# Routed experts on one core: TensorE transposes taken out, rows stored by expert, activations turned on VectorE and through DRAM

## What is computed

```python
kv = np.einsum('bhsd,bhse->bhde', k, v)            # 8 x 8 heads, 576 x 64
out = np.einsum('bhsd,bhde->bhse', q, kv)
x = out / sqrt(mean(out * out, -1) + 1e-6) * g_norm  # -> (4608, 512)

h = x @ w_in                                       # 512 -> 2048
x = (np.maximum(h, 0) + alpha * np.minimum(h, 0)) @ w_out

e_idx = np.argmax(x @ w_gate, axis=1)              # one of 8 experts
gate, eom = softmax(x @ w_gate) at e_idx, sigmoid(x @ w_output_gate) at e_idx
for e in range(8):                                 # w1[e] 512x1024, w2[e] 1024x512
    out[mask] = gate * eom * (np.maximum(x[mask] @ w1[e], 0) @ w2[e])
```

## Time and profile before

| | |
|---|---|
| median of 3 runs | 1506.88 us (1506.14 to 1508.6) |
| the profiled execution's own time | 1503.35 us |
| its span | 1501.5 us |
| instructions | 27268 |
| moved by DMA | 104.51 MB, mean 70 GB/s |

### The profile page before, as it was taken

How to read it: one execution, slowest core, us unless ns; L and a number is a source line. 1 busy time by engine, 2 the same in 40 slices (tenths; PEclk the granted TensorE clock), 3 DMA queues, 4 the chain that set the end, 5 groups by cost and what they waited for, 6 DMA issues and landing times.

```text
span 1501.5 us, 27268 instructions
## 1 busy us (share of the span) xinstructions
PE 1471.3 (98%) x8553; PEld 1280.6 (85%) x8554; DVE 723.3 (48%) x1796; ACT 490.8 (33%) x994; POOL 127.3 (8%) x143
## 2 busy tenths in 40 slices
PE   6899999999999999999999999999999999999997
PEld 6788988888898889898989898887888888888886
DVE  3585555565556565555555555654133114444411
ACT  3343232323232323232232321334233234444422
POOL 1000000000000000000000000112111111111111
PEclk8899999999999999999999999999999999999999
DMA  9242121102121101313000000534133114444411
GB/s 218 82 120 74 33 75 33 43 2 74 33 75 33 43 2 36 70 35 73 23 22 17 6 6 18 118 116 155 44 92 101 46 38 149 154 142 154 149 47 32
DMA packets 100516, 104.51 MB, mean 70 GB/s; under 512 B 55296, under 2 KB 75920, under 8 KB 100434
## 3 DMA queue, kind: packets, MB, share of 16 engines
q1 hardware_dynamic: 91618, 80.99, 19.6%
q0 software_dynamic: 7872, 21.09, 4.4%
q10 hardware_dynamic: 944, 1.33, 0.4%
HBM read 84.04 MB, written 20.65 MB: 70 GB/s over the span
## 4 chain that ended last, share of the span: by engine, by line
PE 91%; DMA 4%; DVE 2%; ACT 1%; issue 1%; POOL 0%; SPq 0%; ACTq 0%; POOLq 0%; DVEq 0%
PE psAcc L1339 25%; PE psH L1327 24%; PE psH L1440 15%; PE psAcc L1461 14%; PE psO L1450 2%; PE psO L1272 2%; PE psO L1242 1%; DMA AR<-in_v_dram 1%; PE psQ L1421 1%; DMA lists<-meta,slot 1%; PE psQ L1258 1%; PE psY L1290 1%; PE psY L1282 1%; DMA AR<-rows,uid 1%; PE psY L1299 1%
## 5 line engine op out<-in xcount | busy, mean ns | idle before, releaser
L1339 PE MATMUL psAcc<-W,XG 128*128 128x512 f32 x1728 | 440.1, 400 | 0.0
L1327 PE MATMUL psH<-XG,W 128*128 128x384 f32 x2304 | 436.3, 337 | 0.7 <-DVE XG L863 0.7
L1327 PEld LDWEIGHTS psH<-XG,W 128*128 128x128 f32 x2304 | 408.6, 188 | 15.5 <-DVE XG L863 0.8
L1339 PEld LDWEIGHTS psAcc<-W,XG 128*128 128x128 f32 x1728 | 314.7, 189 | 66.5 <-issue 5.9
L678 ACT ACTIVATE XG<-AR 128x128 fp32r<-128x128 f32 (+1 forms) x384 | 132.1, 365 | 641.7 <-DVE AR L982 639.5
L979 DVE TENSOR_SCALAR AR<-psH,acol 128x384 f32<-128x384 f32 x192 | 118.4, 617 | 297.3 <-PE psH L1327 297.2
L1440 PE MATMUL psH<-W,XG 128*128 (+1 forms) x996 | 252.0, 402 | 0.0
L1461 PE MATMUL psAcc<-W,XG 128*128 (+1 forms) x984 | 241.8, 394 | 0.0
L1440 PEld LDWEIGHTS psH<-W,XG 128*128 128x128 f32 x996 | 181.7, 189 | 37.3 <-DVE W L960 0.4
L1461 PEld LDWEIGHTS psAcc<-W,XG 128*128 128x128 f32 x984 | 181.7, 188 | 36.8
L1146 DVE TENSOR_TENSOR XG<-psO,XG 128x512 fp32r<-128x512 f32 x82 | 56.6, 690 | 217.8 <-ACT XG L736 217.8
(11 more groups left out here) (200 smaller groups left out, 877.6 us busy)
## 6 DMA issues: line engine op xcount, KB each, us to landing
AR<-in_moe_w_dram SPq DMA_DIRECT2D x68, 512.0 KB, 4.8
AR<-in_k_dram SPq DMA_DIRECT2D x16, 576.0 KB, 5.5
rows<-AR SPq DMA_DIRECT2D x36, 256.0 KB, 2.1
AR<-in_q_dram SPq DMA_DIRECT2D x32, 256.0 KB, 3.1
AR<-in_v_dram SPq DMA_DIRECT2D x14, 576.0 KB, 6.9
AR<-in_moe_w_in_dram SPq DMA_DIRECT2D x16, 256.0 KB, 2.7
AR<-in_moe_w_out_dram SPq DMA_DIRECT2D x16, 256.0 KB, 3.0
AR<-in_v_dram ACTq DMA_DIRECT2D x2, 576.0 KB, 9.5
```

The costliest lines, as they stand in the source:

```text
L1327: mm = pe.matmul(psH[f % 2][:, 0:TILE], w_in_v[:, wp, cc, f * P:(f + 1) * P], xT[:, b, xp, cc, :], start=(cc == 0 and (wp, xp) == PARTS[0] ...
L1339: mm = pe.matmul(psAcc[m][:, :], gT[:, f % 2, gp, m * P:(m + 1) * P], w_out_v[:, wp, f, :], start=(f == 0 and (gp, wp) == PARTS[0]), stop= ...
```

## The change

**Rows.** `rows` and `lists` are gone. For each tile POOL scatters the result rows themselves to `xs` and their two values of gate and token number to `smeta`, in the order of the experts' lists (`put`, six indirect transfers). SP loads the x of a unit in four transfers of 64 KB (`load_x`), 32 partitions each. DVE transposes it in blocks of 32x32 (`x_turn`), ACT and DVE make the two parts from that (`x_high`, `ux_low`).

**h.** DVE transposes each half of h out of PSUM in 32x32 blocks (`h_turn`), SP stores it to the DRAM tensor `hs` (two transfers of 256 KB) and loads it back with the blocks in place (four of 128 KB), ACT applies Relu and writes the high part (`h_high`, two instructions), DVE the low part (`h_low`, four). TensorE does the whole first layer of the next unit before the second layer of this one: `first_layer(u); second(u - 1)`, with two buffers for x and h. The rows of w1 are loaded in another order, and the first layer reads W in runs of 32 columns.

**Weights.** The loads are issued by POOL now. `expert_high` and `expert_low` of a group stand in one piece behind `x_high` and `x_turn`, ahead of `h_high` and `h_turn`.

**The rest.** `block_ends` adds nine small DVE operations and `fill_blocks` nine POOL transfers. The second layer of the very last unit uses parts that ACT and DVE make after the loop (`uhT_last`). In tile 0 the attention of tile 1 moves to steps 4 to 7 (`attention_at`).

```diff
+            def load_x(u, r):
...
+                for c in range(4):
+                    sp.dma_start(xb[32 * c:32 * c + 32, r, :].rearrange("p (t n) -> p t n", t=4),
+                                 xs[bass.ds(at_list, P), c * P:(c + 1) * P].rearrange("(t i) n -> i t n", t=4)
+                                 ).then_inc(x_in[r], 16)
+            def turn_h(u, r):
+                for half in range(2):
+                    sp.wait_ge(uh_flip, 2 * u + half + 2)
...
+                        sp.wait_ge(ut_lo, 4 * u)
+                    sp.dma_start(hs[r, half], hx[half]).then_inc(hs_saved[half], 16)
+                for half in range(2):
+                    sp.wait_ge(hs_saved[half], 16 * u + 16)
...
+                            sp.wait_ge(ut_lo, 4 * u + 4)
+                    for c in range(2):
+                        at_part = 64 * half + 32 * c
+                        sp.dma_start(hb[at_part:at_part + 32, :].rearrange("p (t n) -> p t n", t=4),
+                                     hs[r, half][:, c * 256:(c + 1) * 256].rearrange("(t j) n -> j t n", t=4)
+                                     ).then_inc(hb_in[half], 16)
             # SP, the loop
-                if ahead:
-                    next_ids(u, r, n)
...
+            def unit(u, r, n):
+                load_x(u + 2, r)
+                turn_h(u, r)
+                load_um(u, r, n)
             # POOL, for each tile
+            def put(t):
...
+                for m in range(TG):
+                    pool.indirect_dma_start(xs, bass.IndirectOffsetOnAxis(ap=slot[:, m:m + 1], axis=0),
+                                            y_sb[:, m, :], None).then_inc(placed[m], 16)
             # POOL, the loop
+                first = pool.value_load(tab[0:1, FIRST, bass.ds(u - 1, 1)], min_val=0, max_val=1)
+                with pool.If(first > 0):
+                    turn = pool.value_load(tab[0:1, TURN, bass.ds(u - 1, 1)], min_val=0, max_val=E - 2)
+                    load_expert(pool.value_load(tab[0:1, NEXT, bass.ds(u - 1, 1)], min_val=0, max_val=E - 1),
+                                1, 8 * turn + 12)
...
+                scatter(u - 1, 1 - r)
             # ACT, the loop
+            def unit(u, r, n):
+                x_high(u + 1, 1 - r)
+                group = act.value_load(tab[0:1, GROUP, bass.ds(u - 1, 1)], min_val=0, max_val=2 * E - 1)
                 with act.If(group > 0):
...
+                    for p in range(4):
+                        expert_high(group, p)
+                h_high(u, r)
+                uy(u - 1, 1 - r, n + r)
             # DVE, the loop
-                ut(u, 0)
...
-                ux(u + 1, 1 - r, n + r)
-                group = dve.value_load(tab[0:1, GROUP, bass.ds(u, 1)], min_val=0, max_val=2 * E - 1)
-                split(group, 0)
-                ut(u, 1)
+            def unit(u, r, n):
+                x_turn(u + 1, 1 - r, n + r)
+                group = dve.value_load(tab[0:1, GROUP, bass.ds(u - 1, 1)], min_val=0, max_val=2 * E - 1)
                 with dve.If(group > 0):
...
+                    for p in range(4):
+                        expert_low(group, p)
+                h_turn(u, 0)
+                ux_low(u + 1, 1 - r)
+                h_turn(u, 1)
+                h_low(u, r)
             # TensorE
+            def second(u, r):
+                pe.wait_ge(ut_lo, 4 * u + 8)
+                second_layer(u, uhT[r], *turn_and_parity(u))
...
-                h_transpose(u, 0)
-                h_unit(u, 1)
-                if ahead:
-                    x_units(u + 1, 1 - r, n + r)
-                y_unit(u, 0)
-                h_transpose(u, 1)
-                if ahead:
-                    h_unit(u + 1, 0)
-                y_unit(u, 1)
+            def unit(u, r, n):
+                first_layer(u, r)
+                second(u - 1, 1 - r)
```

More of the change, by code:

```diff
@@ L39 @@
 EPS_RMS, EPS_SUM = 1e-6, 1e-9
-META = 16
 PIECES = ((0, P), (P, TILE))
@@ L310, in over_units @@
                         unit(2 * w + r, r, w)
-            with engine.If(units > UNITS - 1):
-                unit(UNITS - 1, (UNITS - 1) % 2, (UNITS - 1) // 2, ahead=False)
         def load_rows(engine, src, b, half, to, signal):
@@ new lines, in load_expert, with early_expert @@
+            def load_expert(e, half, n):
+                for ch in range(4):
+                    load_piece(e, 4 * half + ch, ch, n + ch)
+            def early_expert(which):
+                return pool.value_load(early[0:1, which:which + 1], min_val=0, max_val=E - 1)
+            for t in range(TILES - 1):
+                put(t)
+            pool.wait_ge(early_set, 4)
+            for n in range(4):
+                load_piece(early_expert(STAR), ORDER[n], n, n)
+            load_expert(early_expert(STAR), 1, 4)
@@ L578, in _ @@
             over_units(pool, units, unit)
+            scatter(units - 1, 0, to=2)
         @block.scalar
@@ L711, in tile @@
                 if before:
-                    act.wait_ge(y_saved, 48 * t)
+                    for m in range(TG):
+                        act.wait_ge(placed[m], 32 * t)
             def expert_high(group, n):
@@ new lines, in split_high, with h_high @@
+            def split_high(to, signal):
+                for p in range(2):
+                    nc.scalar.activation(by_block(to[:, 0, :, :])[:, 2 * p:2 * p + 2, :, :],
+                                         hb_v[:, 2 * p:2 * p + 2, :, :], ACT.Relu).then_inc(signal, 1)
+            def h_high(u, r):
+                for half in range(2):
+                    act.wait_ge(hb_in[half], 32 * u + 32)
+                if not (isinstance(u, int) and u < 2):
+                    act.wait_ge(uy_mm, u)
+                split_high(uhT[r], ut_hi)
@@ new lines, in _ @@
+            x_high(1, 1)
+            for n in range(4):
+                expert_high(1, n)
+            h_high(0, 0)
+            x_high(2, 0)
+            exps(TILES - 1)
+            h_high(1, 1)
+            uy(0, 0, 1)
+            x_high(3, 1)
+            for n in range(4):
+                expert_high(2, n)
+            h_high(2, 0)
+            uy(1, 1, 1)
+            for n in range(4):
+                expert_high(3, n)
+            x_high(4, 0)
+            h_high(3, 1)
+            uy(2, 0, 2)
@@ new lines, in ux_low, with h_turn, split_low @@
+            def ux_low(u, r):
+                dve.wait_ge(ux_hi, u + 1)
+                V.tensor_tensor(uxT[r][:, 1, :], xT32, uxT[r][:, 0, :].bitcast(F32), ALU.subtract).then_inc(ux_lo, 1)
+            def h_turn(u, half):
+                dve.wait_ge(uh_mm, 2 * u + half + 3)
+                if not (isinstance(u, int) and u == 0):
+                    dve.wait_ge(hs_saved[half], 16 * u)
+                V.transpose(out=hx[half], in_=psH[half][:, :]).then_inc(uh_flip, 1)
+            def split_low(to, hi, done, lo):
+                for b in range(4):
+                    if b % 2 == 0:
+                        dve.wait_ge(hi, done + b // 2 + 1)
+                    V.scalar_tensor_tensor(out=by_block(to[:, 1, :, :])[:, b, :, :], in0=hb_v[:, b, :, :], scalar=0.0,
+                                           in1=by_block(to[:, 0, :, :])[:, b, :, :].bitcast(F32),
+                                           op0=ALU.max, op1=ALU.subtract).then_inc(lo, 1)
@@ L1151, in _, with h_low @@
+            def h_low(u, r):
+                split_low(uhT[r], ut_hi, 2 * u, ut_lo)
+            x_turn(0, 0, 0)
+            ux_low(0, 0)
             for n in (2, 3):
                 expert_low(0, n)
+            x_turn(1, 1, 0)
+            ux_low(1, 1)
+            h_turn(0, 0)
+            h_turn(0, 1)
             t = TILES - 1
@@ L1165, in _ @@
                           ).then_inc(lg_set, TG)
-            ux(1, 1, 0)
             pick(t)
-            ut(0, 1)
+            for n in (2, 3):
+                expert_low(1, n)
+            h_low(0, 0)
+            x_turn(2, 0, 1)
+            h_turn(1, 0)
+            ux_low(2, 0)
+            h_turn(1, 1)
             place(t)
-            ut(1, 0)
+            block_ends()
             table_turns()
-            ux(2, 0, 1)
             table_blocks()
-            ut(1, 1)
+            h_low(1, 1)
+            x_turn(3, 1, 1)
+            for n in range(4):
+                expert_low(2, n)
+            h_turn(2, 0)
+            ux_low(3, 1)
+            h_turn(2, 1)
             table_units()
@@ L1401, in side @@
                         x_transpose(a, s - 13)
-                    if not ahead and s == 15:
-                        x_units(0, 0, 0)
                 pe.wait_ge(x_lo, 3 * t + 3)
```

613 lines of the change are left out of this document (261 added, 352 removed).

## The result

The changed kernel takes 1690.74 us (median of 4 runs, 1688.31 to 1696.12) against 1506.51 us for the kernel before beside it. The ratio is 1.1233, with a 95% interval of 1.1212 to 1.1253. The forecast was 1536 in a range of 1490 to 1585: the direction was right, the size far off, 184 us where 29 were forecast.

The account below looks back on a forecast made before the run. TensorE, busy 98% of the span, was taken as the bound. The expert stage at +36 us and tile 0 at -7 gave +29 on 1503.35, 1532.4; with 3.5 for the median, 1536 us, range 1490 to 1585.

Parts of the forecast that it names:

- Tile 0: Dense stage's first tile: moving the attention removes the 6.1 us wait for v and the half clock behind, -7 us (0 to -10).
- Units 0 to 4: Start of the expert stage: 46.4 us of TensorE work remain, plus 5 us (0 to 12) for new waits.
- Pairs: Six pairs of loop bodies with weight groups: weight splits delay the h circle, 15.6 us a pair, 93 in all (66 to 120).
- Plain work: Units without weight groups: TensorE's 10.68 us and the h circle's 10.9 are level, 4 us added over 25 loop bodies.
- The last unit: End of the expert stage: its own parts (0.6 + 1.7 us) are covered by nothing, 2.5 us added.
- Edits at nothing: Edits priced at no cost, among them POOL's row scatter, loads issued on POOL and reading W in runs of 32 columns.
- the contention in the circle: Bodies with a weight group: h's trip through DVE and DRAM meets the next weights, 0.8 us a body (0 to 2.5).
- Rival 2: DVE's transposes become the bound at 1.22 us each instead of 0.69: 12.5 us a plain unit, 1595 us, chance 0.12.
- rival 3: Clock falls after TensorE's holes in bodies with weight groups, or POOL's weights come late: 1558 to 1566 us, chance 0.20.
- Rival 1: The transposes' time comes through: faster if a pair costs below 10.6 us; at 5 a pair 1473 us, chance 0.17.
- the case's own range: Range of the likeliest case, 1498 to 1565 us: pairs at 66 with tile 0 at -10, up to pairs at 120.
- the sign "under 16": A sign that the forecast is wrong: a weight group's body under 16 us; others: plain units above 11.5, v's wait stays.

Follow-up runs that it names:

- w1_plain: The changed kernel with each piece of w1 loaded in plain row order, 128 rows in one run (values not the reference's): 1608.97 us, 1.0693 of the kernel before.
- w1_four: The changed kernel with each 512 KB piece of w1 loaded in four transfers of 32 rows, same row order: 1630.88 us, 1.0844 of the kernel before.
- early_late_2: The changed kernel with w1 in four transfers and all weight splits, in loop and written-out units, moved behind the transposes of h: 1510.9 us, 1.0014 of before.

## Why the prediction was wrong

The end of TensorE's work came at 1679.8 us, 159 behind the 1521 of the forecast's sum. The marks in the trace divide that:

- **Until unit 0**, 1005.7 against 966 (973.3 - 7), 39 us. 18 are the long dense tiles, which no step of mine had and which showed on some chips only. Some 17 are the hole for w1 (1005.7 less 970.6 in `w1_plain`, less the 18). Tile 0 gave 4 instead of 7.
- **Units 0 to 4**: 69.3 us against 52, and 26.8 for the next against 14, 30 in all. `w1_four` took 68.3 and 22.6 there, `early_late_2` 58.4 and 13.4: 5 were w1's source against four transfers (13.5 against the plain order), 19 the splits ahead of the turn, 6 stay. Of the 19, 7.6 are not gained by moving them: in `early_late_2` they come one unit later, 18.7 from unit 5 to unit 6. My 5 for all of this was too small even so.
- **Pairs**: 27.1, 27.9, 27.4, 27.8, 27.4 and 25.8 from the starts of the first layers, 163 against 93, 70 us.
- **Plain work**: 11.15 against 10.68 a unit, 37 x 0.47 = 17, less the 4 allowed, 13.
- **The last unit**: 5.6 of waiting against 2.5, and 7.4 for its second layer at the fallen clock, 5.

**The step that failed** stands in "Edits at nothing": "Loads issued on POOL cost POOL only, unless late". I costed who issues the loads and never the pattern they read. The change says that w1's rows are loaded in another order, and the sum has no term for it. The runs showed that w1's source alone costs the kernel before 110 us. In the changed one it makes w1 land in 13.7 instead of 5.7 us and costs the hole of 17, 13.5 in units 0 to 5 and 29 in the pairs. By total time, 1691 less the 18 of the dense stage is 1673, and `w1_plain` took 1609: an estimate of 64 us, across chips.

**Mis-sized**: the contention in the circle, 0.8 a body, 1.6 a pair. What the bytes add, with and without them, was 9.1 a pair on average, and with w1's source 12.1 (163 less 91, by six); the round trip took 8.5 and 11.5 us, and 8.5 and 14.7 with w1's source, where my sum had 5.8. I had the bound of 2.5 from a weight load among weight loads; a store that waits behind 2 MB and a load behind that store pay twice. The row that would have said so was there: a 256 KB store that took 6.3 instead of 2.1, which I quoted and then didn't use.

**Right**: the place and the mechanism of the pairs (91 against 93 for six without most of the bytes, body 18.97 against 19.0), DVE's prices (0.71, 0.42), the round trip in plain units (4.9 to 5.3 against 5.0), that the splits' place decides (moving them gave 110 us, more than the 91 that the pairs cost without the bytes, so it hides contention too), the direction of tile 0. Rival 2 fell with 0.71 a transpose, and with it the estimate of 1.24 from the Trainium skill (VectorE: DVE Perf Modes, The three transpose paths); DVE's own time is no bound. Of rival 3 the clock came true (after a wait the second layer takes 7.0 to 8.4 instead of 5.6, some 2 us in 12 bodies, part of it hidden), and so did late weights at the end of the dense layer. Rival 1 asked that a pair cost under 10.6: moved splits make it 5.5 to 5.9, and then the transposes' 69 us are still given back. In `early_late_2` TensorE's work alone would end at 973.0 + 46.4 + 400.5 = 1419.9, and it ends at 1502.9, 83 us later: 11.15 instead of 10.68 (17), pairs (35), units 0 to 5 (71.7 against 57 of work, 15), unit 5 to 6 (8), the last unit (9). `early_late_2` at 1.0014 is what is left.

**A slip in the sum**: the lower end of the case's own range, 1498, doesn't follow from the terms named for it. Pairs at 66 and tile 0 at -10 give 1536 - 27 - 3 = 1506. Neither end comes near the measured time.

**The signs**: TensorE waited 165 us for `h_low` and `ux_low` (131.8 + 13.5 + 5.6 + 14.1) where 70 to 110 were forecast, and was busy for 87% of the span, not 90. Bodies with a group took 21.2 to 27.5 us, so the sign "under 16" did not show, nor did the other two: that list had none for a body far above 19.

## What to carry to other kernels

A unit of work that leaves the bound engine comes back as latency: 1.68 us of transposes became a chain over three engines and two trips to DRAM as long as TensorE's own work, so everything else in the loop (weight splits, weight loads) must be placed in the gaps of that chain, not ahead of it. For each transfer that an edit touches, read both access patterns, not the bytes: one whose outermost dimension had 4 steps took 2.4 times as long here (13.7 against 5.7 us), and held up what was issued behind it. And compare variants on one chip only: the same dense code differed here by 18 us between chips.

## What the runs showed of the hardware

- One reordered source, same bytes: landing 5.7 to 13.7 us on POOL's queue, and on SyncE's queue 100 GB/s at 0.2 of the engines.
- With the first layer reading W in runs of 32 columns a unit took 0.27 us more than with adjacent columns (11.15 and 10.88).
- The round trip of 256 KB to DRAM and back in two loads of 128 KB took 4.9 to 5.3 us by itself, 8.5 and 11.5 beside 2 MB of weights, 8.5 and 14.7 with the reordered source.
- A 32x32 block transpose of 128x512 float32 on DVE took 0.71 us, out of PSUM as out of SBUF.
- The same dense code of TensorE took 78.5 us a tile on two chips and 82.4 or 81.0 on others; behind two gaps of 0.9 and 1.1 us the granted clock was 0.58 for 3.6 us. The cause of the gaps is open.
